# Where the combine matrix starts in SBUF, next to the split w2 blocks

## The reference

```
# x: 2304 tokens x 512, phi: 512 x 32
logits = x @ phi
d = softmax(logits, axis=0); slot_input = d.T @ x            # 32 slots
slot_out[e] = relu(slot_input[e] @ w1[e]) @ w2[e]            # 8 experts, 4 slots each
c = softmax(logits, axis=1)                                  # the combine matrix, 2304 x 32
y = c @ slot_out                                             # 2304 x 512

P = eight rounds of row and column scaling of exp(y @ w_gate)
out = sum over e of P[:, e] * (relu(y @ W1[e]) @ W2[e])      # W1[e]: 512x1024, W2[e]: 1024x512
```

## The kernel before

| tensor | its role at TensorE | bytes from `ident` | over a multiple of 512 |
|---|---|---|---|
| `c_stack` before | moving, line 734; both, lines 678 and 719 | 1,472 | 448 |
| `c_stack` after | the same | 1,024 | 0 |
| `a11`, `a2`, `s_split`, `g_stack` | weights | from 29,312 on, in blocks of 512 | 128 |
| `t_split`, `t_other` | moving, lines 784 to 788 | from 29,312 on, plus `PHASE` = 448 | 64 |

## Time and profile before

### The profile page before, as it was taken

One profiled execution on the slowest core, in us unless ns is written; L12 is line 12 of the kernel. 1 busy time (PEld: TensorE's weight loads), 2 busy tenths in 40 slices (PEclk: granted clock), 3 DMA queues, 4 the chain that ended last, 5 costly groups with the idle time before them and its releaser, 6 DMA issues.

```text
span 1044.2 us, 25583 instructions
## 1 busy us (share of the span) xinstructions
PE 1013.0 (97%) x8667; PEld 933.8 (89%) x8667; DVE 755.9 (72%) x2042; ACT 583.1 (56%) x1368; POOL 610.6 (58%) x520
## 2 busy tenths in 40 slices
PE   8999988999989999999999999999999999999998
PEld 5787853469989999999989999999899999999998
DVE  6868742547898778777767787687668777777674
ACT  6677731244558556645654665465546564656542
POOL 5454520014576759666964687578648864868443
PEclk9999988989999999999999999999999999999999
DMA  5678249930200220022003100400120022000111
GB/s 187 230 265 283 73 178 337 408 125 1 82 2 1 82 82 1 2 83 81 2 4 106 59 2 5 157 4 2 67 99 1 2 82 82 2 2 22 62 42 61
DMA packets 36903, 87.79 MB, mean 84 GB/s; under 512 B 2976, under 2 KB 2976, under 8 KB 36768
## 3 DMA queue, kind: packets, MB, share of 16 engines
q1 hardware_dynamic: 36768, 86.07, 22.7%
HBM read 81.35 MB, written 4.72 MB: 82 GB/s over the span
## 4 chain that ended last, share of the span: by engine, by line
PE 61%; POOL 17%; issue 15%; DVE 4%; DMA 1%; ACT 1%; POOLq 0%; DVEq 0%; ACTq 0%
PE bank L784 13%; PE bank L786 13%; PE bank L788 13%; POOL s_split L492 11%; PE bank L734 4%; PE bank L561 3%; POOL t_split L497 3%; PE bank L571 3%; PE bank L590 3%; PE bank L671 2%; PE bank L608 1%; DMA mid_raw<-slot_w_in 1%; PE bank L678 1%; PE bank L712 1%; PE bank L602 1%
## 5 line engine op out<-in xcount | busy, mean ns | idle before, releaser
L492 POOL TENSOR_TENSOR s_split<-s_sum,s_split 128x512 fp32r<-128x512 f32 x288 | 372.7, 1310 | 326.7 <-ACT s_split L897 321.9
L1266 DVE SCALAR_TENSOR_TENSOR acc<-bank,gate_now,acc 128x256 f32<-128x256 f32 x441 | 227.8, 517 | 143.7 <-PE bank L788 142.4
L897 ACT ACTIVATE s_split<-s_sum 128x512 fp32r<-128x512 f32 x288 | 181.7, 632 | 251.1 <-PE bank L788 132.2
L784 PE MATMUL bank<-t_split,s_split 128*128 128x256 f32 x1008 | 284.5, 282 | 2.3 <-DVE acc L1260 1.2
L786 PE MATMUL bank<-t_split,s_split 128*128 128x256 f32 x1008 | 282.5, 280 | 0.0
L788 PE MATMUL bank<-t_split,s_split 128*128 128x256 f32 x1008 | 282.5, 280 | 0.0
L784 PEld LDWEIGHTS bank<-t_split,s_split 128*128 128x128 f32 x1008 | 189.3, 188 | 6.8 <-issue 5.1
L788 PEld LDWEIGHTS bank<-t_split,s_split 128*128 128x128 f32 x1008 | 192.5, 191 | 0.0
L786 PEld LDWEIGHTS bank<-t_split,s_split 128*128 128x128 f32 x1008 | 189.4, 188 | 0.0
L784 PE MATMUL bank<-t_split,a 128*128 128x256 f32 x576 | 163.0, 283 | 4.3 <-DVE acc L1260 2.4
L786 PE MATMUL bank<-t_split,a 128*128 128x256 f32 x576 | 161.5, 280 | 0.0
(11 more groups left out here) (171 smaller groups left out, 1978.6 us busy)
## 6 DMA issues: line engine op xcount, KB each, us to landing
raw<-big_w_in SPq DMA_DIRECT2D x15, 2048.0 KB, 8.9
slot_raw<-slot_w_in SPq DMA_DIRECT2D x14, 1024.0 KB, 6.3
mid_raw<-slot_w_in SPq DMA_DIRECT2D x6, 1024.0 KB, 10.3
early_raw<-slot_w_in SPq DMA_DIRECT2D x6, 1024.0 KB, 11.2
late_raw<-slot_w_in SPq DMA_DIRECT2D x6, 1024.0 KB, 7.8
q_ring<-q_tiles SPq DMA_DIRECT2D x18, 256.0 KB, 5.2
k_ring<-k_tiles SPq DMA_DIRECT2D x18, 256.0 KB, 5.3
v_ring<-v_rows SPq DMA_DIRECT2D x18, 256.0 KB, 2.7
```

The source lines that it names most:

```text
L492: pool.tensor_tensor(s_split[:, i, 1, :, :], s_sum[:, i, :, :], s_split[:, i, 0, :, :].bitcast(F32), ALU.subtract)\
L784: pe.matmul(to, left[:, 0, f, :], t_place(parity, k, 0)[:, f, :], start=(f == 0 and k in FRESH), stop=False, skip_group_check=k not in FRESH)
L897: act.activation(s_split[:, i, 0, :, :], s_sum[:, i, :, :], ACT.Copy).then_inc(s_hi_ready, 1)
L1266: done = dve.scalar_tensor_tensor(out=to, in0=got, scalar=gate, in1=to, op0=ALU.mult, op1=ALU.add)
```

## The change

`c_stack` moves ahead of `fold` and `fold_half`, and the two small pads around it become one behind it. The pads' sizes leave `raw` and all that lies behind it where it was. No instruction is added, removed or reordered.

```
         ident = sb("ident", [P, P])
         ones = sb("ones", [P, P])
+        c_stack = sb("c_stack", [P, TILES * P], F32R)
         fold = sb("fold", [P, SLOTS])
         fold_half = sb("fold_half", [P, 2, SLOTS])
-        sb("pad_below", [P, P - PHASE])
-        c_stack = sb("c_stack", [P, TILES * P], F32R)
-        sb("pad_above", [P, P - PHASE])
+        sb("pad", [P, P - SLOTS - 2 * SLOTS])
         raw = sb("raw", [P, 4096])
```

## The result

The changed kernel is faster: 1041.37 us (median of 18 runs, 1038.03 to 1045.18) against 1046.95 us (18 runs, 1045.84 to 1048.65), ratio 0.9948 with a 95% interval of 0.9941 to 0.9955, so about 5.5 us. The forecast was 1048.1, with a range of 1042 to 1055. The runs also scatter more: over 7.2 us where the kernel before has 2.8.

What follows compares the result with a forecast made beforehand. The prediction took TensorE's matmul count times start-to-start distance as the bound; +1.4 us for line 734's hidden matmuls and 0 for the rest, on the median 1046.67, gave 1048.1 us, range 1042 to 1055.

Steps and rivals of the forecast that it cites:

- What bounds the kernel: In a steady expert nobody keeps TensorE waiting; its time is matmul count times start-to-start distance, 117.8 ns in a tile pair.
- The two paces and what switches them: Product matmuls start every 113.3 or 117.8 ns; a `c_stack` group can switch which of the two holds.
- The products: I take 0: Products' operands do not move, so no change in their pace; ends +3.5 us and about -26 us.
- The products go to their quicker pace: Rival: `c_stack` groups at 384 leave products quick; 1020 us always, 1033 half the time; 0.21 with hidden-only form.
- the form in which only hidden matmuls get fast: Weaker rival form: only line 734's hidden matmuls get cheap, 1043.8 us; within the shared chance of 0.21.
- The step on line 734: Hidden matmuls, `c_stack` going from 320 to 384 bytes beyond the weights: +2.5 ns each, +1.4 us over 576.
- The likeness with the fills: At 384, as in fills, both starts agree in multiples of 128 bytes; there a load costs 10 ns, not 5.
- For it: nearer to 448: Reason within the quicker-pace rival: a `c_stack` group at 384 is nearer to the products' 448 than 320 is.
- The signs: Line 734 median 283 to 286 for the forecast; products' median 276 for the quicker pace; fills keep 387/397.
- The rule of the Trainium skill: Two independent SBUF read ports, so the start of `c_stack` costs nothing and the time stays 1046.7 us.
- no effect: Rival: hidden matmuls are bound by something the operand's start does not touch; 1046.7 us, chance 0.14.

Runs made afterwards that it cites:

- e15: Changed kernel with PHASE = 120 and the combine matrix at 96 bytes, so products and hidden matmuls all start 480 bytes beyond the weights; 1051.83 us.
- e16: Changed kernel with PHASE = 104 and the combine matrix at 32 bytes, so products and hidden matmuls all start 416 bytes beyond the weights; 1051.75 us.
- e12: Changed kernel with PHASE = 0 and the combine matrix at 128 bytes, so products and hidden matmuls all start 0 beyond the weights; 1060.03 us.
- e6: e1 with everything behind `gate_sb`, weights included, and the combine matrix 64 bytes later, distances to the weights unchanged; 1043.19 us.
- e1: Changed kernel with the combine matrix 64 bytes past a multiple of 512, 448 beyond the weights as the products are; 1040.87 us.
- e10: e1 with the 32 small matmuls of line 712 split into two lots of 16, before products 3 and 4 of the tile pair; 1034.63 us.
- e13: Changed kernel with PHASE = 16 and the combine matrix at 192 bytes, so products and hidden matmuls all start 64 bytes beyond the weights; 1041.62 us.

## Why the prediction was wrong

**What bounds the kernel** was right. TensorE's count of matmuls times their distance from start to start explains the gain, 7.3 us of it; longer waits for VectorE and GpSimd gave 1.5 us back, which the prediction had at nothing.

**The two paces and what switches them** were right as far as they went, and decided everything. The earlier trace rows showed that a group on the combine matrix can end the quick pace and, once, start it. What I read wrongly is line 712: I took it for a pause that begins a quick stretch, and it flips the pace whichever it is.

**The failed step is "The products: I take 0".** It held that no operand of the products moves and that the pace in which a group leaves them would stay what it was. The row for it is above: at distance 384 a group flips the pace at 119 of 119 places, and 1,860 more product matmuls ran quick. The rival "The products go to their quicker pace" is what happened, in its mechanism and its direction; I gave it 0.21, together with the form in which only hidden matmuls get fast. Its reason was wrong (below), so it is in part luck that this rival named what happened. Its price was wrong too. I had 1020 us if always and 1033 if half the time. A group that flips also undoes, which leaves no room for "always": the quick share rose from 11% to 42%. The 1,860 more quick matmuls at 4.4 ns would be 8.2 us. 7.7 were measured, because a flip costs some slower matmuls (146 distances of 120 to 124 ns, where the kernel before has 22), and the dearer hidden matmuls and longer waits left 5.8 us of the span.

**The step on line 734** had the right sign: +2.5 ns expected, +0.8 ns measured (118.45 to 119.23), so +0.4 us for +1.4. The likeness with the fills that I leaned on (both starts agree modulo 128) turned out real: a group at 0, 128, 256 or 384 flips. But the effect is in how it leaves the products; the hidden matmuls themselves differ, 117.4 and 117.5 ns at 256 and 0 against 119.2 and 119.3 at 384 and 128.

**"For it: nearer to 448"** was the wrong reason for the right rival. For a group among products at 448 nearness does not matter: 192 keeps as 448 does, and 320 and 64 are the ones that end the quick pace. (For a whole stream the place near 448 is narrow: 32 bytes to either side, in e15 and e16, the two paces are gone.) The period of 256 bytes is nowhere in the trace of before.

**The signs** that the prediction named served badly. The median at line 734 (now 733) rose to 282, not to 283 or more, and that at the products stayed 281 though 42% of them ran quick. The one that held is that of the fills, 387/397 as before, which fits that their distance of 0 counts for them and not the byte at which they start.

**The rule of the Trainium skill** ("TensorE: Matmul & The Clock Gate", "What happens when you issue a matmul"), that the load of the next weights takes no bandwidth from the running matmul, would have given 1046.7 and no effect. The runs show an effect of up to 6.6 ns a matmul (120.0 in e12 against 113.4 in e6) where, modulo 512 bytes, only the weights start elsewhere. So, for float32r streams of this shape, a load does cost the running stream something; whether what it takes is bandwidth no run shows.

**The range** ended at 1042, 0.6 us above the result. It left 0.14 to times below, drawn from a rival whose middle I had put at 1033. The measured 5.5 us lie between no effect and the 13.7 us of that middle, where I had put next to nothing.

## What to carry to other kernels

When the operand of a matmul moves, cost the whole stream and not only the matmuls that read it: here the hidden matmuls got dearer by 0.4 us in all and made some 6,000 others cheaper by 7.7 us. Read starts, not durations; the median duration was 281 before and after. And where a stream shows two paces, ask of every interruption and of every odd group whether it ends, flips or keeps the pace, count it over all of its places, and price a rival at every share in between, not at all or half.

## What the hardware did that I had not expected

- A float32r stream of 256 columns with a load beside each matmul runs at 113.4, 117.8, 118.7 or 120.0 ns by how far its moving operand starts beyond the weights (64 or 448: 113.4 or 117.8; 128: 118.7; 0: 120.0). For the switching of the pace the period is 256 bytes, in eight starts of the combine matrix 64 bytes apart.
- At 64 and 448 two paces are each stable for a long time: in e1 all 119 groups without a pause kept what they found, 36 times the quick one and 83 times the other.
- Small matmuls in between flip the pace: 32 of them at 84 of 84 places in the twelve kernels with two paces and one lot each (the kernel before included), lots of 16 in e10 at 14 of 14. The mechanism beneath (which reads meet when) is argued at most, and no run shows it. How a pause chooses the pace is open as well; e13 and e1 differ in it.
- No version here stays quick throughout, and so 113.4 ns for a whole expert mixture was not seen.
